# The second phase's first product by one Strassen level: seven block products for eight

## What is computed

```python
kv = einsum('bhsd,bhse->bhde', k, v)              # q, k, v: 8 batches, 8 heads, 576 rows, 64 columns
o = einsum('bhsd,bhde->bhse', q, kv)
x = o / sqrt(mean(o * o) + 1e-6) * g_norm         # heads put side by side: (8, 576, 512)

h = maximum(x @ w_in, 0)                          # first gated layer; w_in (512, 1024)
u, v = h[..., :512], h[..., 512:]
v_n = (v - mean(v)) / sqrt(var(v) + 1e-6)
v_s = einsum('ts,bsd->btd', w_spatial, v_n) + b_spatial[None, :, None]
x = (u * v_s) @ w_out                             # (512, 512)

h = maximum(x @ w_in2, 0)                         # second layer; w_in2 (512, 1024)
conv = sum over k of conv_w[k] * h shifted by k - 1 rows
out = (h * sigmoid(conv)) @ w_out2                # w_out2 (1024, 512); out (8, 576, 512)
```

## Time and profile before

| | us |
|---|---|
| median of 3 runs | 820.81 (820.35 to 822.75) |
| the profiled execution | 822.27 |
| its span in the trace | 820.5 |
| PE busy, share of the span | 807.3, 98% |
| DVE busy | 467.8, 57% |
| ACT busy | 386.3, 47% |
| POOL busy | 39.7, 5% |
| granted clock of PE, mean | 0.997 of full speed |

### The profile page before, as it was taken

The page is one execution under the profiler, slowest core; times in us unless marked ns, Lnnn a source line. Parts: engine busy times, 40 slices in busy tenths (PEclk is TensorE's granted clock), DMA queues, the critical chain, the costliest instruction groups (busy, mean ns, idle before and its releaser), DMA issues.

```text
span 820.5 us, 15569 instructions
## 1 busy us (share of the span) xinstructions
PE 807.3 (98%) x6102; PEld 729.1 (89%) x6102; DVE 467.8 (57%) x945; ACT 386.3 (47%) x674; POOL 39.7 (5%) x44
## 2 busy tenths in 40 slices
PE   8998999999999999999999999999999999999998
PEld 7668989797988989798999898999989899898996
DVE  3876574665567475657368183481825728166470
ACT  3664352634345262533547283463725637265461
POOL 2342000000000000000230000000000000000000
PEclk9999999999999999999999999999999999999999
DMA  9872324535241443322020301203012020120001
GB/s 312 291 247 58 142 92 116 173 87 192 70 169 66 122 159 91 127 73 101 15 103 1 109 1 38 85 1 109 2 51 70 5 103 0 51 71 26 26 0 64
DMA packets 24661, 74.29 MB, mean 91 GB/s; under 512 B 2386, under 2 KB 2610, under 8 KB 20660
## 3 DMA queue, kind: packets, MB, share of 16 engines
q1 hardware_dynamic: 24484, 73.84, 27.3%
q10 hardware_dynamic: 144, 0.01, 0.0%
HBM read 54.84 MB, written 19.00 MB: 90 GB/s over the span
## 4 chain that ended last, share of the span: by engine, by line
PE 92%; DVE 4%; DMA 1%; ACT 1%; issue 0%; SPq 0%; DVEq 0%; ACTq 0%
PE ps L385 51%; PE ps L547 24%; PE ps L416 11%; PE ps L336 2%; PE ps L352 2%; DMA kv_raw<-kv_rest_dram 1%; PE ps L364 1%; PE ps L486 1%; DVE x_gated_split L893 0%; DVE vrr L918 0%; DVE work L925 0%; PE ps L474 0%; DVE bn_stats L905 0%; DVE v_hg_split L931 0%; DVE w_product_split L993 0%
## 5 line engine op out<-in xcount | busy, mean ns | idle before, releaser
L385 PE MATMUL ps<-x_gated_split,w_product_split 128*128 128x288 f32 x1536 | 204.8, 294 | 0.0
L385 PEld LDWEIGHTS ps<-x_gated_split,w_product_split 128*128 128x128 f32 x1536 | 204.3, 188 | 0.5
L547 PE MATMUL ps<-w_in_split,v_hg_split 128*128 128x512 f32 x832 | 194.6, 389 | 0.0
L547 PEld LDWEIGHTS ps<-w_in_split,v_hg_split 128*128 128x128 f32 x832 | 155.7, 188 | 32.0
L1035 DVE SCALAR_TENSOR_TENSOR work<-work,const_cols 128x576 f32<-128x576 f32 x64 | 52.4, 819 | 151.4 <-ACT work L785 151.3
L385 PE MATMUL ps<-w_sp_split,v_hg_split 128*128 128x288 f32 x896 | 121.7, 297 | 2.4 <-DVE w_sp_split L954 2.4
L385 PEld LDWEIGHTS ps<-w_sp_split,v_hg_split 128*128 128x128 f32 x896 | 120.8, 190 | 2.6 <-issue 2.6
L385 PE MATMUL ps<-x_gated_split,w_in_split 128*128 128x288 f32 x768 | 104.3, 296 | 1.1 <-ACT work L638 1.1
L385 PEld LDWEIGHTS ps<-x_gated_split,w_in_split 128*128 128x128 f32 x768 | 102.2, 188 | 3.2 <-ACT work L638 1.6
L416 PE MATMUL ps<-w_in_split,x_gated_split 128*128 128x512 f32 x384 | 93.5, 396 | 1.3 <-DVE kv_double L849 0.8
L416 PEld LDWEIGHTS ps<-w_in_split,x_gated_split 128*128 128x128 f32 x384 | 70.4, 188 | 22.1 <-issue 7.4
(11 more groups left out here) (96 smaller groups left out, 691.4 us busy)
## 6 DMA issues: line engine op xcount, KB each, us to landing
kv_raw<-kv_main_dram SPq DMA_DIRECT2D x8, 2048.0 KB, 9.0
q_raw<-q_T_dram SPq DMA_DIRECT2D x8, 1152.0 KB, 5.1
gated_scratch<-work SPq DMA_DIRECT2D x32, 288.0 KB, 2.1
q_raw<-gated_scratch SPq DMA_DIRECT2D x8, 1152.0 KB, 5.7
out_dram<-o_x SPq DMA_DIRECT2D x32, 256.0 KB, 2.0
sq_then_r<-r_scratch SPq DMA_DIRECT2D x14, 576.0 KB, 6.2
kv_raw<-kv_rest_dram SPq DMA_DIRECT2D x8, 256.0 KB, 9.1
work<-w_in_dram SPq DMA_DIRECT2D x2, 1024.0 KB, 15.0
```

Of the source, the lines that this page charges most:

```text
L385: last = pe.matmul(pair[bank][:, c, :], st, mo[:, c * HALF:(c + 1) * HALF], start=(n == 0), stop=(n == len(steps) - 1))
L547: last = pe.matmul(PS[:, ROW_BANK[i], :], x, wout2[:, w, f, :], start=(f == 0 and n == 0), stop=(f == FT - 1 and n == len(PASSES) - 1))
```

## The change

In the second phase the gated batch X (512 by 576, transposed) and W are cut in two by two blocks, and the product is formed by one level of Strassen's method in the Winograd form, with seven block products for eight:

- **Weights.** W is kept unsplit (`W_copy` on ACT in the start-up; the eight `W_lo` of DVE are gone) and is split at the end of the first phase. There DVE's `combine_weights` forms four sums of blocks (128x1024 each) and seven LO parts, ACT's `weight_hi` seven HI parts. They stand between the last `v_lo` and `gate` 0 of the last batch.
- **Operands.** In the first phase DVE forms four differences of X's blocks for each batch (`t_block`, 128x576 each) behind the last gate. SP stores three blocks of X (288 KB each) and the four differences in one DMA of 1152 KB (`store_gated`). In the second phase SP loads seven operand blocks, 2016 KB in two DMAs, once the batch before has made its last in-product; ACT and DVE split each (`operand_hi`, `operand_lo`, seven each of 128x576 for four of two tiles' size before).
- **In-products.** `in_product(b, g, k)`: 4 groups g by 7 products k, each 6 matmuls of 128x288 into one of 8 PSUM banks in turn. Product number n = 7g + k waits until bank n mod 8 has been read.
- **Sums.** For each g one copy on ACT (`first_copy`, 128x288) and seven additions on DVE (128x288, one input from PSUM) give h's tiles g and g + 4. `h_relu` then works in place from SBUF.
- **Order of the tiles.** The turns take the tiles in the order 4, 0, 5, 1, 6, 2, 7, 3 (`F_ORDER`). All eight h tiles have a buffer of their own.
- **Out product.** It goes tile by tile: for each tile e, when its h_lo is there, 3 matmuls for each of the four row tiles. The four row tiles are evicted at the end, each into its own buffer, behind the next batch's seven `operand_hi` on ACT.

The core of the diff:

```diff
+PRODUCTS = [(A11, B11), (S2, T2), (A12, B21), (S3, T3), (S1, T1), (A22, T4), (S4, B22)]
+LAST_SUM = [None, 0, 1, 2, 4, 5, 6]
+F_ORDER = [4, 0, 5, 1, 6, 2, 7, 3]
+TOP_SUM, LOW_SUM = 6, 5
...
-            def store_gated(b, m0, m1):
-                for m in range(m0, m1):
-                    sp.wait_ge(s_g, b * MT + m + 1)
-                    sp.dma_start(gated_dram[b, m], u_sb[m]).then_inc(s_go[m], DMA)
...
+            def store_gated(b):
+                for n, (ready, blk, k, l) in enumerate(((2, B11, 0, 0), (4, B21, 1, 0), (4, B22, 1, 1))):
+                    sp.wait_ge(s_g, b * MT + ready)
+                    sp.dma_start(op_dram[b, blk].rearrange("p (j t) -> p j t", j=2), gated(k, l)).then_inc(s_go[n], DMA)
+                sp.wait_ge(s_T, (b + 1) * 4)
+                sp.dma_start(op_dram[b, T2:T4 + 1].rearrange("k p t -> p k t"),
+                             TB[:, :].rearrange("p (k t) -> p k t", k=4)).then_inc(s_To, DMA)
...
-                        sp.wait_ge(s_gt, (2 * p + c + 1) * 2)
-                        load_gated(2 * p + c + 1)
+                        sp.wait_ge(s_in, (2 * p + c + 1) * PER_BATCH)
+                        load_operands(2 * p + c + 1)
...
+            def in_product(b, g, k, pairs):
+                n = g * NPROD + k
+                first = isinstance(b, int) and b == 0
+                if g == 0:
+                    pe.wait_ge(s_oplo, b * NPROD + k + 1)
+                if n == 0:
+                    if first:
+                        pe.wait_ge(s_Slo, NPROD)
+                        pe.wait_ge(s_g, B * MT - 1)
...
+                if n == 2 and first:
+                    pe.wait_ge(s_g, B * MT)
...
+                if n >= 8:
+                    g0, k0 = divmod(n - 8, NPROD)
+                    if k0 == 0:
+                        pe.wait_ge(s_x1, b * GROUPS + g0 + 1)
+                    else:
+                        pe.wait_ge(s_sum, b * PER_BATCH + g0 * NPROD + LAST_SUM[k0] + 1)
...
+                steps = [(weight[a][:, w, j, g * P:(g + 1) * P], operand[o][:, x, j * HALF:(j + 1) * HALF]) for j in (0, 1) for w, x in PASSES]
...
+                for e in range(FT):
+                    pe.wait_ge(s_hlo, b * FT + e + 1)
+                    for i in range(FULL):
+                        last = rows_product(i, e)
...
+            def body2(b, odd, ahead):
+                first_copy(b, 0)
+                for e in range(FT + 2):
+                    if e < FT:
+                        h_relu(b, e)
+                        tap1(b, e)
+                    if e >= 2:
+                        h_hi(b, odd, e - 2)
+                    if 0 <= e - 1 < FT:
+                        sigmoid(b, e - 1)
+                    if e + 1 < GROUPS:
+                        first_copy(b, e + 1)
+                if ahead:
+                    for k in range(NPROD):
+                        operand_hi(b + 1, k)
...
+            act.wait_ge(s_To, DMA * B)
...
+                dve.wait_ge(s_To, DMA * b)
+                t_block(b, T1, gated(0, 1), gated(0, 0))
+                t_block(b, T3, gated(1, 1), gated(0, 1))
...
+            def add(b, g, dst, x, k, product):
+                dve.wait_ge(s_in, b * PER_BATCH + g * NPROD + product + 1)
+                dve.tensor_tensor(dst, x, PS[:, (g * NPROD + k) % 8, 0:HALF], ALU.add).then_inc(s_sum, 1)
...
             def body2(b, odd, ahead):
...
+                sums_a(b, 0)
+                sums_b(b, 0)
+                sums_c(b, 0)
+                for e in range(FT + 2):
+                    g = e + 1
+                    if g < GROUPS:
+                        sums_a(b, g)
+                    if e < FT:
+                        tap0(b, e)
+                    if g < GROUPS:
+                        sums_b(b, g)
+                    if e >= 2:
+                        h_lo(b, odd, e - 2)
+                    if e < FT:
+                        tap2(b, e)
+                    if g < GROUPS:
+                        sums_c(b, g)
+                    if 0 <= e - 1 < FT:
+                        mul(b, e - 1)
```

More of the change, by code:

```diff
@@ L581, in run @@
-                for f in range(FT):
-                    last = rows_product(FULL, f)
+                pe.wait_ge(s_sum, (2 * p + 2) * PER_BATCH)
+                for e in range(FT):
+                    last = rows_product(FULL, e)
                 last.then_inc(s_rout, 1)
@@ L769, in _ @@
             body(B - 1, False)
[L770 to L771 removed]
+            for k in range(NPROD):
+                operand_hi(0, k)
             act.wait_ge(s_wo2_in, DMA)
[L773 removed]
+            for f in F_ORDER:
                 act.activation(wout2[:, HI, f, :], wo2_raw[:, f, :], ACT.Copy).then_inc(s_wo2_hi, 1)
[L777 to L780 removed]
@@ L795, in h_hi, with sigmoid @@
+            def sigmoid(b, e):
+                act.wait_ge(s_conv, b * FT + e + 1)
+                act.wait_ge(s_hlo, b * FT + max(e - 1, 0))
+                act.activation(p_sb[e % 2], t_sb[e % 2], ACT.Sigmoid).then_inc(s_sig, 1)
+            def h_hi(b, odd, e):
+                act.wait_ge(s_mul, b * FT + e + 1)
+                if e == 0:
                     act.wait_ge(s_out, b * FULL)
+                if e == 4 and isinstance(b, int) and b == 0:
+                    act.wait_ge(s_wo2, FT)
@@ L822, in run @@
                         act.wait_ge(s_rout, p)
-                    for _ in body2(b, odd):
-                        if not (last and odd):
-                            gated_hi(b + 1, 0)
-                            gated_hi(b + 1, 1)
+                    body2(b, odd, not (last and odd))
                 act.wait_ge(s_rout, p + 1)
@@ L955, in body @@
                                       ALU.subtract).then_inc(s_b, 1)
+                if not ahead:
+                    combine_weights()
                 gate(b, 0)
@@ L1013, in _ @@
             x_scale(0, 1)
-            W_lo(3)
             x_lo(0, 0)
@@ L1054, in body2 @@
             def body2(b, odd, ahead):
-                for f in range(FT + 2):
-                    if f < FT:
-                        tap0(b, f)
-                    if f >= 2:
-                        h_lo(b, odd, f - 2)
-                    if f < FT:
-                        tap2(b, f)
-                    if 0 <= f - 1 < FT:
-                        mul(b, f - 1)
-                if ahead:
-                    gated_lo(b + 1, 0)
-                    gated_lo(b + 1, 1)
-            for s in s_go:
-                dve.wait_ge(s, DMA * B)
@@ L1071, in _ @@
+                if ahead:
+                    for k in range(NPROD):
+                        operand_lo(b + 1, k)
+            for i in range(FT):
                 dve.memset(h_sb[i][:, 0:1], 0.0)
```

429 lines of the change are left out of this document (254 added, 175 removed).

## The result

| | before | after |
|---|---|---|
| median of the runs compared, us | 821.5 (820.35 to 822.75) | 842.37 (841.8 to 843.05) |
| ratio | | 1.0253 [1.0241, 1.0266] |
| profiled execution; its span | 822.27; 820.5 | 841.8; 840.0 |
| granted clock, mean | 0.997 | 0.992 |

What follows compares the result with a forecast made beforehand. PE's work was taken as the bound before, and PE waiting for h_lo after. -1.6 start-up + 13.1 between the phases + 0.5 second batch + 3 x 0.47 pairs = +13.4, so 834.2 us; forecast 827 to 841, range 820 to 846.

Steps and rivals of the forecast that it cites:

- The walk through a batch: Second-phase loop: waits followed in order; last h_lo at t = 43.9 in an even batch, PE waiting for h_lo.
- dear sums: Rival, second-phase additions: 0.54 us each instead of 0.45, a pair 102.6, the kernel 843 us; chance 0.11.
- Pairs: Second-phase loop: two batches cost 100.4 us for 99.88 before, counted as 3 x 0.47 for three pairs.
- Second batch: Second phase, the batch after the first: 0.5 us more.
- Between the phases: From first phase to second: late gate 3, differences and their store lose 13.1 us, once.
- The same stretch along PE: PE between the phases: waits of 0.8, 3.4 and 6.0 us, twenty products left, out product's end at 477.2.
- the clock: Rival, second-phase loop: gaps each batch lower PE's clock, 8 x 1.6 = 13 us, the kernel 847; chance 0.07.
- gate 3's gap: Between the phases: PE's third product waits for gate 3 and loses 3.4 us.
- the store's gap: Between the phases: PE stands 6.0 us, since ACT may not begin before the differences are stored.
- Start-up: Start of the kernel: without DVE's eight W_lo, PE saves its waits, about 1.6 us.
- PE stays the bound: Rival, second-phase loop: PE never waits, a pair costs 93.5 us, the kernel 807; chance 0.13.
- POOL beside DVE: Between the phases: POOL's w_out2 split stretches DVE operations with two SBUF inputs, taken as 1.1 us each; PSUM-input sums not stretched.

Runs made afterwards that it cites:

- x1_apart: The changed kernel with ACT's first_copy tiles in memory of their own, not waiting for the store of the differences; 836.95 us, 1.0181 of before.
- reordered: The changed kernel with new orders of DVE's and ACT's second-phase programs, same operations and waits; 811.23 us, 0.9870 of before.
- transition: The changed kernel with first_copy tiles apart, gate 3 before the last four operand splits, POOL's w_out2 split behind the differences; 831.38 us, 1.0109 of before.

## Why the prediction was right, and where its size fell short

The direction, the places of the loss and the range of 820 to 846 held. The forecast of 834.2 was 8.2 us low, and the measured time lies 1.4 us over the narrower 827 to 841. By its own steps:

- **The walk through a batch.** It held to a few tenths. On the time axis of the batch that starts at 633.08, DVE enters turn 1 at 12.8 (645.91; forecast 12.8), turn 3's tap0 starts at 25.4 (658.47; forecast 25.3), the last h_lo ends at 44.2 (677.26; forecast 43.9 in an even batch, and this is one). An addition cost 0.45 as taken, so the dear sums of 0.54 are out; DVE's 39.1 us are 38.5 and 40.6. The idle time of PE that `h_lo` ends, forecast as 3 us a batch, is 13.9 / 8 = 1.7; about as much again stands inside the longer matmuls.
- **Pairs, +1.4 forecast, +4.8 measured.** A pair is 101.56 for 100.4. The even batch takes 47.74 for 47.15, the odd one 53.82 for 47.8 + 5.45 = 53.25. Each part was a little short: 28 products at 0.80 instead of 0.795 (0.15 a batch), a turn 2.98 even and 3.07 odd (the rows of 12 matmuls at 3.06 in the chain) instead of 2.96, and 0.8 instead of 0.55 between the last h_lo and the end of the 12 matmuls behind it. Some 0.6 us on a batch of 50 is a good walk, but the forecast gain or loss per pair was only the small difference between two large numbers, 100.4 - 99.88, so it was wrong by a factor of three. (The sum also took 0.47 a pair where the walk gives 0.52; that is 0.15 us in all.)
- **Second batch, +0.5 forecast, +1.0 measured.** It is an odd batch, and the same term.
- **Between the phases, 11.5 with the start-up forecast, 13.7 measured.** Its mechanisms all showed, with other sizes. The times here have the start-up's 1.6 taken off the forecast's. The path goes by DVE and the store: gate 3 ends at 423.5 for 421.0, and the four differences at 429.8 for 425.5 (+4.3), since beside POOL a split took 1.77 us and a difference 1.6 where I took 1.1 for each. That is the term that was mis-sized. The store took 4.4 us for 5.7, so ACT's first copy begins at 434.5 for 431.4 (+3.1). From there to the second batch it is 477.82 - 434.47 = 43.35 for 44.2 (-0.9). The sum is +2.2.
- **The same stretch along PE, and the clock.** Here the in-products begin at 417.0 for 416.0 (+1.0), gate 3's gap is 5.03 for 3.4 (+1.6), the six products between the gaps take 7.0 for 4.8 (+2.2), the store's gap is 4.31 for 6.0 (-1.7), the last twenty products take 17.7 for 15.9 (+1.8), and from there it is 25.2 for 27.9 (-2.7), which is +2.2 again. This reading shows a term that was left out, the clock: from start to start the products behind the first gap took 1.57, 1.44, 1.42 and then 0.80 us, behind the second 1.61, 1.44, 0.92 and then 0.80, so PE lost 2.0 + 1.6 = 3.6 us to it. I had put the clock down as a rival for the loop, with the rows that show it, and not asked the same of the two large gaps of my own forecast. Here that cost the forecast next to nothing (0.2 us by the comparison with x1_apart), since the end of batch 0 hangs on the copy.
- **Start-up.** The w_spatial product of the first batch starts at 75.66 for 77.01: 1.35 us gained for 1.6. The two waits that the earlier trace rows shows make 1.3 of it; for the further 0.3 no row stood.
- **The rivals.** *PE stays the bound* didn't happen, but its price was right: reordered has just this loop, at 93.84 us a pair for my 93.5. I gave as the reason against it that the tail is a chain of waits and "leaves no room"; that holds for the order as written, not for the work. *The clock*, as a rival for the loop, is out: its windows stand at 1.00, so PE's idle times of about 1 us there didn't lower it. The Trainium skill, in TensorE: Matmul & The Clock Gate (A second HAM failure mode: psum-queue depth-cycling), tells of short idle gaps between groups of matmuls that make the clock swing; no row of this loop shows it.
- **POOL beside DVE.** The GPSIMD Engine Reference of the Trainium skill (1. Specifications) was followed for what is stretched, two SBUF inputs, and not for how much. The gate with a PSUM input took 0.74 us beside POOL, as elsewhere; a split took 1.77 for 0.70. The Trainium skill, in SBUF — State Buffer (Terms), says that the port pair is locked for a whole instruction and the loser waits. The trace agrees with that: one of POOL's splits is 13.55 / 8 = 1.69 us, and DVE gets about one operation through in that time. By it, the seven operations would have been 7 x 1.7 = 11.9 us, an estimate; they took 5.32 + 2.72 + 3.59 = 11.6. That the additions would not be stretched, `transition` shows: beside POOL the first five of group 0 in a row took 1.90 us, as in x1_apart without POOL. Of the `tap` operations with two SBUF inputs that ran beside POOL there, one took 1.42 us and two 0.81 as elsewhere. So one operation for each of POOL's is what an unbroken row of them showed, and not every single one.

## What to carry to other kernels

When a product gets cheaper by moving work to another engine, compare volumes first (here 39 of 47 us: it fits), but then walk the waits in the order in which the two static programs are written; where the walk shows an engine idle on both sides in turn, try other orders in the same walk before dropping the idea, for here the order alone was worth 31 us of 842 and the sign of the result. Where a phase boundary becomes a chain, list every engine that works there, the one "off the path" too: POOL's eight splits, hidden before, cost 6.5 us once DVE's splits stood beside them on the path. And a gap of PE of several us in a forecast has two prices, its idle time and the clock behind it, but ask first what the end of the stretch hangs on: here it hung on the start of one copy, and a gap of 5.03 us with 2.0 us of slow products behind it cost nothing.

## What the hardware showed beyond that

- The clock stood at 0.50 with the first matmul behind gaps of 5.03 and 4.31 us. In `transition` PE stood 2.80 us before the out product, and the 12 matmuls behind it took 2.98 us at a granted clock of 1.00, while before had a gap of 2.40 with 0.56 behind it. In x1_apart a gap of only 2.12 us at the same place had 0.50 behind it (window 449 to 451). The length of one gap alone doesn't tell whether the clock falls. Nor does it fall at one point: in after it was down while PE still stood (0.55 from 421 to 423), in before a microsecond after the matmuls had begun again (1.00 from 76 to 78, 0.56 from 78 to 80). The timeline row of `transition` and the window on it:

```profile
443.17 2.98 PE L624 MATMUL ps<-w_in_split,v_hg_split 128*128 128x512 f32 x12 [2.80 <-DVE v_hg_split L1221]
```

```profile
443.00:445.00 2.00, 1.83 (x8) 1.57 (x9) 2.00 (x5) 0.00 (x0) 0.00 (x0) 1.00 1.04 411
```

- A matmul stream that waits a little for each tile shows as longer matmuls and waiting weight loads, not as idle PE: in after 84 matmuls took 20.6 us in one piece where they need 19.1, and the page calls PE 96% busy. The weight loads' idle time tells of it sooner than PE's share: it is 66.0 us at L622, 33.5 of it ended by `h_lo`, where the same loads stood 32.0 us in before and 32.2 in reordered.
